# Seven products of halves in place of eight for x times w_in in the last three steps of an attention and two-layer gated kernel

## Chip, cores and metric

The kernel runs on one core of one Trainium2 chip. The metric is device time in microseconds (us), lower is better. The time before is 1128.55 us, the median of 3 runs (1128.35 to 1129.04).

## What is computed

```python
scores = scale * np.matmul(q, k.transpose(0, 1, 3, 2))           # 4 batches x 8 heads, 576 x 64
thresh = np.max(scores, axis=-1, keepdims=True) - tau
scores = np.where(scores >= thresh, scores, -1000000000.0)
attn = softmax(scores)                                           # row max, exp, sum + 1e-9
x = np.matmul(attn, v)  ->  2304 tokens x 512
h = x @ w1_in;  x = (h * clip(h + 3, 0, 6) / 6) @ w1_out         # w_in 512 x 2048, w_out 2048 x 512
h = x @ w2_in;  out = (h / (1 + exp(-1.702 * h))) @ w2_out
```

All arrays are float32. The matmuls run on fp32r operands, each operand split in a high and a low part, and each product is the sum of three: high times high, high times low, low times high.

## The kernel before

The engines are written out by hand, each with its own program and semaphores; nothing schedules them. After the attention the work falls into four steps: step 0 and 1 are the first layer with the first and the second half of the 2048 hidden columns, step 2 and 3 the second layer in the same way. A step 1 or 3 adds to the partial sums that the step before it left in HBM.

Step 0 goes over eight tiles of 288 tokens. The first six are mixed piece by piece into the attention of the next batch (`mixed_piece`); tiles 6 and 7 come behind it (`MIXED` is 6), and this stretch is called the seam below. Steps 1 to 3 go over six tiles of 384 tokens each. A tile has two parts on TensorE (PE):

- `h_chunk` (L526): eight chunks of 128 hidden columns. A chunk sums over `KC` = 4 blocks of 128 rows of w_in, three matmuls a block, so 12 matmuls of 128x384 a chunk and 96 a tile. The chunks go round four PSUM banks (`h_bank`, shown as `mm` and `tr`); chunk c waits until chunk c-4 is read.
- `y_chunk` (L535 in step 1, L537 in steps 2 and 3): the gated h times w_out. Four blocks of 24 matmuls of 128x384 in step 1, three blocks of 24 matmuls of 128x512 in steps 2 and 3, in four other banks (`y_bank`, shown as `score`).

For each h chunk ScalarE (ACT) makes the gate from the bank (L800 Relu of h + 3, or L803 Sigmoid), VectorE (DVE) multiplies it with the bank into `act_f` (L680, L682), ACT rounds that into `g_hi` (L808), and GpSimd (POOL) takes the difference, `g_lo` (L963). For x, ACT makes `x_hi` (L795) and DVE `x_lo` (L672). For the weights of the next step, 512 KB a unit, ACT makes `w_hi` (L787) and POOL `w_lo` (L953); these have two buffers and are made in the tiles of the step before. Every transfer is issued by SyncE (SP), in its own fixed order. At the seam ACT and POOL also split the first eight weight units of step 1 (`SEAM`, `SEAM_SLOTS`).

## Time and profile before

| | |
|---|---|
| median of 3 runs | 1128.55 us |
| the profiled execution | 1127.87 us, span 1126.0 us |
| attention with the first six tiles of step 0 | up to 475.8 us |
| tiles 6 and 7 of step 0 | 475.8 to 526.9 us |
| steps 1, 2, 3 | 526.9 to 726.6, to 924.7, to 1122.9 us |
| busy: PE, DVE, ACT, POOL | 96%, 50%, 49%, 43% |

The page gives busy times and the chain of work that ended last; the trace is asked for groups of instructions, stretches of time and single engines. Durations of one instruction are in ns, times in a stretch in us. Matmuls overlap in the pipeline, so the pace of PE is read from the chain (so many matmuls in so many us), not from the duration of one.

### The profile page before, as it was taken

The page shows a single profiled execution, that of the slowest core. Times are in us where ns is not written, and L with a number is a line of the kernel's source. Part 1 is how long each engine was busy: PE and PEld are TensorE (multiplying, and loading weights), DVE is VectorE, ACT ScalarE, POOL GpSimd, SP SyncE. Part 2 cuts the span into 40 slices and gives each one's busy share as a digit, 9 for nine tenths or more (in the row PEclk, how much of TensorE's full clock was granted, in tenths as well). Part 3 has the DMA queues.
Part 4 walks back from the last instruction along what each step waited for, and adds up shares of the span by engine and source line. Part 5 has one row for each costly group of instructions (what it writes and reads, how often), then busy time and mean ns, then how long its engine had stood idle before and what let it go on. Part 6 is the DMA issues. An engine that isn't in the chain of part 4 may idle for free.

```text
span 1126.0 us, 17711 instructions
## 1 busy us (share of the span) xinstructions
PE 1084.6 (96%) x6720; PEld 1021.7 (91%) x6720; DVE 559.6 (50%) x1040; ACT 549.4 (49%) x1036; POOL 487.7 (43%) x582
## 2 busy tenths in 40 slices
PE   4888899999999999999999999999999999999998
PEld 3676799999999999999999999989999889999987
DVE  5989878887878887433233222223322222332221
ACT  4888876868686866344334322333322223332221
POOL 3566755545545553384544332144333122222222
PEclk9999999999999999999999999999999999999999
DMA  4447453445343622463233322112221101222210
GB/s 123 118 138 187 118 135 109 122 120 140 111 121 87 169 85 78 115 182 127 89 106 122 122 84 84 41 54 94 94 94 57 56 28 57 85 85 84 84 57 28
DMA packets 91044, 112.37 MB, mean 100 GB/s; under 512 B 25536, under 2 KB 69712, under 8 KB 90960
## 3 DMA queue, kind: packets, MB, share of 16 engines
q1 hardware_dynamic: 90656, 110.96, 33.8%
q8 instruction: 53, 0.87, 0.3%
q10 hardware_dynamic: 304, 0.30, 0.1%
q14 instruction: 31, 0.25, 0.1%
HBM read 78.12 MB, written 33.10 MB: 99 GB/s over the span
## 4 chain that ended last, share of the span: by engine, by line
PE 90%; DVE 4%; issue 3%; ACT 2%; DMA 0%; POOL 0%; SPq 0%; ACTq 0%; POOLq 0%
PE mm L526 20%; PE score L537 17%; PE tr L526 14%; PE score L535 12%; PE score L488 7%; PE tr L503 6%; PE mm L535 6%; PE mm L517 6%; DVE prob L648 2%; DVE neg_max L640 1%; DVE pt_lo L666 1%; ACT pt_hi L775 1%; ACT gate L800 0%; DMA q_raw<-in_qT 0%; ACT prob L770 0%
## 5 line engine op out<-in xcount | busy, mean ns | idle before, releaser
L963 POOL TENSOR_TENSOR g_lo<-act_f,g_hi 128x384 fp32r<-128x384 f32 (+1 forms) x208 | 196.5, 950 | 405.2 <-ACT g_hi L808 405.2
L526 PE MATMUL mm<-x_hi,w_hi 128*128 128x384 f32 (+1 forms) x512 | 162.9, 318 | 0.6 <-DVE x_lo L672 0.5
L526 PE MATMUL mm<-x_hi,w_lo 128*128 128x384 f32 (+1 forms) x512 | 162.2, 317 | 0.0
L526 PE MATMUL mm<-x_lo,w_hi 128*128 128x384 f32 (+1 forms) x512 | 162.1, 317 | 0.0
L775 ACT ACTIVATE pt_hi<-tr 128x640 fp32r<-128x640 f32 x144 | 101.7, 706 | 98.3 <-PE tr L503 97.8
L803 ACT ACTIVATE gate<-mm 128x384 f32<-128x384 f32 x48 | 23.7, 494 | 220.6 <-PE mm L526 220.6
L488 PE MATMUL score<-k_hi,q_sp 128*128 128x288 f32 x320 | 97.7, 322 | 29.3 <-DVE prob L648 20.6
L666 DVE TENSOR_TENSOR pt_lo<-tr,pt_hi 128x640 fp32r<-128x640 f32 x144 | 118.1, 820 | 9.8 <-ACT pt_hi L775 8.8
L640 DVE TENSOR_REDUCE neg_max<-score 128x1 f32<-128x576 f32 x144 | 108.2, 752 | 27.4 <-PE score L488 24.3
L933 POOL TENSOR_SCALAR thresh<-neg_max,tau_abs 128x1 f32<-128x1 f32 x144 | 41.6, 289 | 178.6 <-DVE neg_max L640 178.0
L648 DVE SCALAR_TENSOR_TENSOR prob<-score,thresh,prob 128x576 f32<-128x576 f32 x144 | 116.2, 807 | 0.0
L503 PE MATMUL tr<-ident,prob 128*128 128x128 f32 x720 | 105.2, 278 | 7.6 <-issue 5.3
L537 PE MATMUL score<-w_lo,g_hi 128*128 128x512 f32 x288 | 112.3, 390 | 0.0
L537 PE MATMUL score<-w_hi,g_lo 128*128 128x512 f32 x288 | 112.2, 390 | 0.0
L537 PE MATMUL score<-w_hi,g_hi 128*128 128x512 f32 x288 | 112.0, 389 | 0.0
L770 ACT ACTIVATE prob<-score,neg_max 128x576 f32<-128x576 f32 x144 | 106.4, 739 | 7.8 <-DVE neg_max L640 7.5
L808 ACT ACTIVATE g_hi<-act_f 128x384 fp32r<-128x384 f32 (+1 forms) x208 | 102.7, 494 | 7.3 <-DVE act_f L680 4.7
L526 PE MATMUL tr<-x_hi,w_hi 128*128 128x384 f32 (+1 forms) x320 | 105.7, 330 | 0.0
L526 PE MATMUL tr<-x_lo,w_hi 128*128 128x384 f32 (+1 forms) x320 | 105.6, 330 | 0.0
L526 PE MATMUL tr<-x_hi,w_lo 128*128 128x384 f32 (+1 forms) x320 | 105.6, 330 | 0.0
L503 PEld LDWEIGHTS tr<-ident,prob 128*128 128x128 f32 x720 | 83.1, 142 | 18.1 <-issue 17.1
L488 PEld LDWEIGHTS score<-k_hi,q_sp 128*128 128x128 f32 x320 | 62.0, 194 | 40.9 <-DVE prob L648 31.1
(82 smaller groups left out, 2463.6 us busy)
## 6 DMA issues: line engine op xcount, KB each, us to landing
x_raw<-x_t_scratch SPq DMA_DIRECT2D x18, 768.0 KB, 6.3
q_raw<-in_qT SPq DMA_DIRECT2D x64, 144.0 KB, 2.8
k_raw<-in_kT SPq DMA_DIRECT2D x62, 144.0 KB, 2.9
stage<-in_w_in SPq DMA_DIRECT2D x16, 512.0 KB, 7.0
stage<-in_w_out SPq DMA_DIRECT2D x16, 512.0 KB, 5.5
o_parts_scratch<-o_t SPq DMA_DIRECT2D x32, 160.0 KB, 1.8
x_t_scratch<-x_raw SPq DMA_DIRECT2D x8, 576.0 KB, 3.4
part_t_scratch<-y_out SPq DMA_DIRECT2D x8, 576.0 KB, 3.5
```

What stands on the lines that cost most here:

```text
L488: m = pe.matmul(score[:, g % 2, half, 0:HALF], q_sp[:, col:col + P], k_part[:, side, half * HALF:half * HALF + HALF], start=e == 0, stop=e ...
L503: m = pe.transpose(turned_p[:, c * P:c * P + P], prob[:, x % PROBS, c * P:c * P + P], ident[:, :])
L526: m = pe.matmul(bank[:, 0:width], w[:, col:col + P], x[:, k, 0:width], start=(k == 0 and e == 0), stop=(k == KC - 1 and e == 2))
L535: r = pe.matmul(bank[:, 0:width], w[:, col + m * P:col + m * P + P], g[:, c, 0:width], **ends)
L537: r = pe.matmul(bank[:, :], g[:, c, m * P:m * P + P], w[:, col:col + DM], **ends)
L640: dve.tensor_reduce(neg_max[:, r:r + 1], score[:, g % 2, :, 0:HALF], AX.XY, ALU.max, negate=True).then_inc(max_done, 1)
L648: dve.scalar_tensor_tensor(out=p, in0=score[:, g % 2, :, 0:HALF], scalar=thresh[:, r:r + 1], in1=p, op0=ALU.is_ge, op1=ALU.mult, accum_out ...
L666: dve.tensor_tensor(pt_place(pt_lo, x), turned_place(x), pt_place(pt_hi, x), ALU.subtract).then_inc(pt_lo_done, 1)
L770: act.activation(prob[:, g % PROBS, 0:S].rearrange("p (a n) -> p a n", a=2), score[:, g % 2, :, 0:HALF], ACT.Exp, bias=neg_max[:, r:r + 1] ...
L775: act.activation(pt_place(pt_hi, x), turned_place(x), ACT.Copy).then_inc(pt_hi_done, 1)
L808: act.activation(g_hi[:, c, 0:width], act_f[:, c % 2, 0:width], ACT.Copy).then_inc(g_hi_done, 1)
L963: pool.tensor_tensor(g_lo[:, c, 0:width], act_f[:, c % 2, 0:width], g_hi[:, c, 0:width], ALU.subtract).then_inc(g_lo_done, 1)
```

## The change

Attention and step 0 keep their instructions. In steps 1 to 3, two tiles of 384 tokens are taken together as a pair (three pairs a step, `d` = 0 to 8). The pair's x is cut in halves by token and by row of w_in, w_in in halves by row and by column, and the four quarters of h are formed from seven products of such halves or of their sums and differences (`PRODUCT`), where the plain way has eight. One product is 6 matmuls of 128x384 (two blocks of 128 rows, three each). The hidden columns of a step go in four groups of two chunks (n and n + 4), so a group is seven products and gives four quarters ("items" C11, C12, C21, C22), and the products go round six banks (`p_bank`).

The four items of a group are summed from the seven banks: ACT copies the first product into `sum12`, and DVE adds the other six in seven additions, each with one operand in SBUF and one in a bank, into `sum11`, `sum12`, `sum21`, `sum22`. ACT makes the gate from the sum into a ring of three places (`act_ring`), DVE multiplies it in place with the sum (both in SBUF, `gate_item`), ACT rounds (`high_item`), POOL subtracts (`low_item`). An ACT gate waits until POOL is done with the item three before it.

The sums of halves of x (4 pieces a pair) are made and split on DVE and ACT behind a pair's products, for the next pair (`bring`). The sums of halves of w_in (8 units a step) are made and split on DVE, ACT and POOL behind the products of a step's last pair, for the next step. w_out has one buffer now; its eight chunks are split in a step's first pair, two behind the first item of each of its four groups, by ACT (`high_out_unit`) and POOL (`low_out_unit`). The second part keeps its matmuls; its blocks run over the two tiles of a pair, the first three blocks leave out the last group until all three have the other groups (`dense_block`). SP loads x in pieces of 192 columns, w_in in rows of 128 columns, and stores and loads y by block. The first w_in units of step 1, their sums included, are made at the seam. SBUF places are given by hand, and buffers of the attention are reused.

```diff
+    PAIR_TILES = NTOK // (2 * TT)
+    DENSE = (STEPS - 1) * PAIR_TILES
+    HIGH_A = ("A11", "A22", "A12", "S3", "S2", "S1", "S4")
+    HIGH_B = ("B11", "B22", "B21", "T3", "T1", "T2", "T4")
+    PRODUCT = {1: ("A11", "B11"), 2: ("A12", "B21"), 3: ("S4", "B22"), 4: ("A22", "T4"), 5: ("S1", "T1"),
+               6: ("S2", "T2"), 7: ("S3", "T3")}
+    PRODUCT_ORDER = (1, 2, 6, 7, 5, 3, 4)
+    GROUPS = FC // 2
+    PRODUCTS = GROUPS * len(PRODUCT_ORDER)
+    BANKS = 6
...
+    ITEMS = [(0, "C11")]
+    for n in range(1, GROUPS):
+        ITEMS += [(n - 1, "C22"), (n - 1, "C12"), (n - 1, "C21"), (n, "C11")]
+    ITEMS += [(GROUPS - 1, "C22"), (GROUPS - 1, "C12"), (GROUPS - 1, "C21")]
...
+        def coming(d):
+            if d + 1 == DENSE:
+                return []
+            x = [("x", 4 * max(d + 1, 0) + i) for i in range(4)]
+            units = unit_of(1, 0, 0) if d < 0 else next_units(d)
+            if units is None:
+                return [x[0:2], x[2:4]]
+            w = [("w", units + i) for i in range(2 * GROUPS)]
+            if d < 0:
+                return [x[2:4], w[4:6], w[6:8]] if d == -1 else [w[2:4]]
+            return [x[0:2], w[0:2], x[2:4], w[2:4], w[4:6], w[6:8]]
+        def emptied_behind(d):
+            if d < 0:
+                return [1, 2, 3]
+            if next_units(d) is None:
+                return [3, 5] if blocks_y(d) == 8 else [2, 4]
+            return [0, 2, 4, 5, 6, 7] if blocks_y(d) == 8 else [0, 1, 3, 4, 5, 5]
...
+            def product(d, n, k):
+                p = PRODUCT_ORDER[k]
+                a, b = HIGH_A.index(PRODUCT[p][0]), HIGH_B.index(PRODUCT[p][1])
+                bank = p_bank[(len(PRODUCT_ORDER) * n + k) % BANKS][:, 0:TT]
+                for j in range(2):
+                    for e, (w, x) in enumerate(((ws_hi, xs_hi), (ws_hi, xs_lo), (ws_lo, xs_hi))):
+                        m = pe.matmul(bank, w[:, n, j, b, :], x[j][:, a, :], start=j == 0 and e == 0, stop=j == 1 and e == 2)
+                m.then_inc(made, 1)
...
+            def bank_free(d, n, k):
+                at = len(PRODUCT_ORDER) * n + k
+                if at >= BANKS:
+                    m, i = divmod(at - BANKS, len(PRODUCT_ORDER))
+                    if i == 0:
+                        pe.wait_ge(p1_copied, GROUPS * d + m + 1)
+                    else:
+                        pe.wait_ge(evicted, 6 * (GROUPS * d + m) + i)
...
+            for d in range(DENSE):
+                for n in range(GROUPS):
+                    units_split(pe, dense_step(d), 0, n)
+                    if n == 0:
+                        pe.wait_ge(pair_split, 4 * (d + 1))
+                    for k in range(len(PRODUCT_ORDER)):
+                        bank_free(d, n, k)
+                        product(d, n, k)
+                for b in range(3):
+                    dense_block(d, b, 0, GROUPS - 1)
+                for b in range(3):
+                    dense_block(d, b, GROUPS - 1, GROUPS)
+                for b in range(3, blocks_y(d)):
+                    dense_block(d, b, 0, GROUPS)
...
+            def pair_sums(q):
+                a21, a11, a22, a12 = (pair_raw[:, q % 2, i, :] for i in range(4))
+                dve.wait_ge(pair_lo_done, q + 1)
+                dve.tensor_tensor(a22, a21, a22, ALU.add).then_inc(pair_s1_done, 1)
+                dve.tensor_tensor(a21, a11, a21, ALU.subtract).then_inc(pair_s1_done, 1)
+                dve.wait_ge(pair_s1_done, 3 * q + 2)
+                dve.tensor_tensor(a11, a22, a11, ALU.subtract).then_inc(pair_s1_done, 1)
+                dve.wait_ge(pair_s1_done, 3 * q + 3)
+                dve.tensor_tensor(a12, a12, a11, ALU.subtract).then_inc(pair_sums_done, 1)
...
+            def gate_item(d, n, which, bank):
+                k = item(d, n, which)
+                place = act_ring[:, k % 3, :]
+                dve.wait_ge(gate_done, k + 1)
+                if dense_step(d) == 1:
+                    r = dve.scalar_tensor_tensor(out=place, in0=place, scalar=6.0, in1=bank, op0=ALU.min, op1=ALU.mult)
+                else:
+                    r = dve.tensor_tensor(place, place, bank, ALU.mult)
+                r.then_inc(gated_done, 1)
+            def evict(d, n, k):
+                dve.wait_ge(made, PRODUCTS * d + len(PRODUCT_ORDER) * n + k + 1)
+                return p_bank[(len(PRODUCT_ORDER) * n + k) % BANKS][:, 0:TT]
+            def add_c11(d, n):
+                bank = evict(d, n, 1)
+                dve.wait_ge(p1_copied, GROUPS * d + n + 1)
+                dve.tensor_tensor(sum11[:, :], sum12[:, n % 2, :], bank, ALU.add).then_inc(evicted, 1)
+            def add_u2(d, n):
+                place = sum12[:, n % 2, :]
+                dve.tensor_tensor(place, place, evict(d, n, 2), ALU.add).then_inc(evicted, 1)
+            def add_u3(d, n):
+                bank = evict(d, n, 3)
+                dve.wait_ge(evicted, 6 * (GROUPS * d + n) + 2)
+                dve.tensor_tensor(sum21[:, :], sum12[:, n % 2, :], bank, ALU.add).then_inc(evicted, 1)
+            def add_c22_u4(d, n):
+                bank, place = evict(d, n, 4), sum12[:, n % 2, :]
+                dve.wait_ge(evicted, 6 * (GROUPS * d + n) + 3)
+                dve.tensor_tensor(sum22[:, :], sum21[:, :], bank, ALU.add).then_inc(c22_added, 1)
+                dve.tensor_tensor(place, place, bank, ALU.add).then_inc(evicted, 1)
+            def add_c12(d, n):
+                bank, place = evict(d, n, 5), sum12[:, n % 2, :]
+                dve.wait_ge(evicted, 6 * (GROUPS * d + n) + 4)
+                dve.tensor_tensor(place, place, bank, ALU.add).then_inc(evicted, 1)
+            def add_c21(d, n):
+                dve.tensor_tensor(sum21[:, :], sum21[:, :], evict(d, n, 6), ALU.add).then_inc(evicted, 1)
...
+            for d in range(DENSE):
+                first_of_step = d % PAIR_TILES == 0
+                for n in range(GROUPS + 1):
+                    if n > 0:
+                        gate_item(d, n - 1, "C22", sum22[:, :])
+                        gate_item(d, n - 1, "C12", sum12[:, (n - 1) % 2, :])
+                        gate_item(d, n - 1, "C21", sum21[:, :])
+                    if n < GROUPS:
+                        add_c11(d, n)
+                        add_u2(d, n)
+                        gate_item(d, n, "C11", sum11[:, :])
+                        add_u3(d, n)
+                        add_c22_u4(d, n)
+                        add_c12(d, n)
+                        add_c21(d, n)
+                empty = 0
+                for two, many in zip(coming(d), emptied_behind(d)):
+                    bring(two)
+                    if two[0][0] == "x":
+                        bring_low(two)
+                    while empty < many:
+                        empty_block(d, empty)
+                        empty += 1
+                    if two[0][0] == "w":
+                        bring_low(two)
+                for b in range(empty, blocks_y(d)):
+                    empty_block(d, b)
...
+            for d in range(DENSE):
+                first_of_step = d % PAIR_TILES == 0
+                for n in range(GROUPS + 1):
+                    if n > 0:
+                        act.wait_ge(evicted, 6 * (GROUPS * d + n - 1) + 5)
+                        gate_of(d, n - 1, "C12", sum12[:, (n - 1) % 2, :])
+                        act.wait_ge(evicted, 6 * (GROUPS * d + n))
+                        gate_of(d, n - 1, "C21", sum21[:, :])
+                    if n < GROUPS:
+                        copy_p1(d, n)
+                    if n > 0:
+                        high_item(d, n - 1, "C22")
+                        high_item(d, n - 1, "C12")
+                    if n < GROUPS:
+                        act.wait_ge(evicted, 6 * (GROUPS * d + n) + 1)
+                        gate_of(d, n, "C11", sum11[:, :])
+                    if n > 0:
+                        high_item(d, n - 1, "C21")
+                    if n < GROUPS:
+                        high_item(d, n, "C11")
+                        if first_of_step:
+                            high_out_unit(dense_step(d), 2 * n)
+                            high_out_unit(dense_step(d), 2 * n + 1)
+                        act.wait_ge(c22_added, GROUPS * d + n + 1)
+                        gate_of(d, n, "C22", sum22[:, :])
+                for two in coming(d):
+                    bring(two)
...
+            for d in range(DENSE):
+                if d == 0:
+                    pool.wait_ge(y_stored, 16 * TILES)
+                for k in range(len(ITEMS)):
+                    low_item(d, k)
+                    if d % PAIR_TILES == 0 and k % 4 == 0 and k < 4 * GROUPS:
+                        low_out_unit(dense_step(d), k // 2)
+                        low_out_unit(dense_step(d), k // 2 + 1)
+                for two in coming(d):
+                    bring(two)
```

The first place is DVE's program in a group of a pair (step 1): before, for four chunks of a tile, and now, for four items. In the names, sum_104 is sum11, sum_106 sum12, sum_103 sum21, sum_105 sum22.

```order
L680 SCALAR_TENSOR_TENSOR act_f<-gate,mm 128x384 [waits g_lo_done,gate_done] x2
L680 SCALAR_TENSOR_TENSOR act_f<-gate,tr 128x384 [waits g_lo_done,gate_done] x2
```

```order
L1038 SCALAR_TENSOR_TENSOR act_ring<-act_ring,sum_105 128x384 [waits gate_done]
L1038 SCALAR_TENSOR_TENSOR act_ring<-act_ring,sum_106 128x384 [waits gate_done]
L1038 SCALAR_TENSOR_TENSOR act_ring<-act_ring,sum_103 128x384 [waits gate_done]
L1051 TENSOR_TENSOR sum_104<-sum_106,tr 128x384 [waits p1_copied,made]
L1055 TENSOR_TENSOR sum_106<-sum_106,score 128x384 [waits made]
L1038 SCALAR_TENSOR_TENSOR act_ring<-act_ring,sum_104 128x384 [waits gate_done]
L1060 TENSOR_TENSOR sum_103<-sum_106,score 128x384 [waits evicted,made]
L1065 TENSOR_TENSOR sum_105<-sum_103,score 128x384 [waits evicted,made]
L1066 TENSOR_TENSOR sum_106<-sum_106,score 128x384
L1071 TENSOR_TENSOR sum_106<-sum_106,mm 128x384 [waits evicted,made]
L1074 TENSOR_TENSOR sum_103<-sum_103,mm 128x384 [waits made]
```

Four instructions became eleven, and the multiplication with the gate of C11 stands ahead of the additions that free the next banks.

The second place is POOL's program at the start of step 1: before, the splits of the last seam units between the first tile's g_lo, and now, the first pair's items and chunks of w_out.

```order
L963 TENSOR_TENSOR g_lo<-act_f,g_hi 128x384 [waits g_hi_done] x4
L953 TENSOR_TENSOR w_lo<-stage,w_hi 128x512 [waits w_hi_done] x4
L963 TENSOR_TENSOR g_lo<-act_f,g_hi 128x384 [waits g_hi_done] x8
```

```order
L1530 TENSOR_TENSOR gd_lo<-act_ring,gd_hi 128x384 [waits g_hi_done,y_stored]
L1522 TENSOR_TENSOR wo_lo<-unit_raw_89,wo_hi 128x512 [waits wo_hi_done]
L1522 TENSOR_TENSOR wo_lo<-unit_raw_90,wo_hi 128x512 [waits wo_hi_done]
L1530 TENSOR_TENSOR gd_lo<-act_ring,gd_hi 128x384 [waits g_hi_done] x4
L1522 TENSOR_TENSOR wo_lo<-unit_raw_89,wo_hi 128x512 [waits wo_hi_done]
```

Two splits of w_out stand between the items of each of the first pair's groups, and the very first item waits for the last store of step 0.

The third place is ACT's program at the start of tile 6, at the seam: before, and now.

```order
L787 ACTIVATE w_hi<-stage 128x1024 [waits pt_lo_done,inv_stored1,pv_done,inv_stored0,stage_loaded0,o_stored1,o_stored0]
L787 ACTIVATE w_hi<-stage 128x1024 [waits stage_loaded1]
L800 ACTIVATE gate<-mm,three 128x288 [waits mm_filled] x2
```

```order
L1263 ACTIVATE ws_hi<-unit_raw_89 128x384 [waits pt_lo_done,inv_stored1,pv_done,inv_stored0,unit_loaded0,o_stored1,o_stored0]
L1268 ACTIVATE ws_hi<-unit_raw_89 128x512 [waits unit_sums_done]
L1263 ACTIVATE ws_hi<-unit_raw_90 128x384 [waits unit_loaded1]
L1268 ACTIVATE ws_hi<-unit_raw_90 128x512 [waits unit_sums_done]
L1236 ACTIVATE gate<-mm,three 128x288 [waits mm_filled] x2
```

Ahead of tile 6's first gates, ACT now twice waits for sums that DVE makes behind a split on POOL.

## Rows read from the trace of the kernel before

**Rows 1.** The page: busy time of the engines, clock granted to PE by slice

```profile
PE 1084.6 (96%) x6720; PEld 1021.7 (91%) x6720; DVE 559.6 (50%) x1040; ACT 549.4 (49%) x1036; POOL 487.7 (43%) x582
...
PEclk9999999999999999999999999999999999999999
```

**Rows 2.** Stretches: seam, steps 1, 2, 3; length, busy by engine, clock, DMA

```profile
460.47:527.00 66.53, 66.46 (x504) 66.02 (x503) 21.18 (x43) 25.80 (x54) 39.76 (x43) 1.00 0.47 134
527.00:726.58 199.58, 199.58 (x1153) 199.58 (x1152) 55.28 (x96) 69.40 (x131) 74.49 (x68) 1.00 0.28 97
726.58:924.71 198.13, 198.13 (x1009) 181.04 (x1009) 55.14 (x90) 61.68 (x128) 69.94 (x64) 1.00 0.21 70
924.71:1126.00 201.29, 198.16 (x1009) 180.73 (x1007) 53.25 (x87) 52.43 (x116) 48.44 (x48) 1.00 0.22 71
```

**Rows 3.** The chain that ended last, steps 1 and 2: start, us, what

```profile
597.62 4.16 PE tr L526 x24
...
610.10 16.64 PE score L535 x96
...
743.22 16.36 PE score L537 x72
759.58 4.18 PE mm L526 x24
```

**Rows 4.** Groups by shape, DVE and ACT: busy us, mean ns, idle before

```profile
L682 DVE TENSOR_TENSOR act_f<-gate,mm 128x384 f32<-128x384 f32 x48 | 26.6, 554 | 78.3 <-ACT gate L803 78.3
...
L635 DVE TENSOR_TENSOR k_lo<-k_raw,k_hi 128x576 fp32r<-128x576 f32 x1 | 0.8, 758 | 0.0
...
L803 ACT ACTIVATE gate<-mm 128x384 f32<-128x384 f32 x48 | 23.7, 494 | 220.6 <-PE mm L526 220.6
...
L800 ACT ACTIVATE gate<-mm,three 128x384 f32<-128x384 f32 x24 | 14.0, 582 | 99.5 <-PE mm L526 99.4
...
L808 ACT ACTIVATE g_hi<-act_f 128x384 fp32r<-128x384 f32 x144 | 74.8, 519 | 4.0 <-DVE act_f L682 2.5 <-DVE act_f L680 1.5
```

**Rows 5.** Groups by shape, POOL

```profile
L963 POOL TENSOR_TENSOR g_lo<-act_f,g_hi 128x384 fp32r<-128x384 f32 x144 | 145.2, 1014 | 382.2 <-ACT g_hi L808 382.2
...
L953 POOL TENSOR_TENSOR w_lo<-stage,w_hi 128x512 fp32r<-128x512 f32 x64 | 83.6, 1330 | 18.4 <-ACT w_hi L787 18.4
```

**Rows 6.** All x_lo on DVE, both inputs in SBUF: min/median/max ns

```profile
L672 DVE TENSOR_TENSOR x_lo<-x_raw,x_hi x104: 435/547/1312, 113.2 to 1077.8; 128x384 fp32r<-128x384 f32 x72, 128x288 fp32r<-128x288 f32 x32
```

**Rows 7.** One such x_lo run and the POOL work beside it, in order of time

```profile
645.59 2.72 DVE L672 TENSOR_TENSOR x_lo<-x_raw,x_hi 128x384 fp32r<-128x384 f32 x4 [1.01 <-ACT x_hi L795]
...
644.49 1.99 POOL L963 TENSOR_TENSOR g_lo<-act_f,g_hi 128x384 fp32r<-128x384 f32 x2 [1.06 <-ACT g_hi L808]
```

**Rows 8.** The seam in order of time: chain, then ACT, DVE, POOL

```profile
475.78 3.40 PE mm L526 x24
...
501.51 3.16 PE mm L526 x24
...
477.79 1.06 ACT L787 ACTIVATE w_hi<-stage 128x1024 fp32r<-128x1024 f32 x1 [2.65 <-DMA stage<-in_w_in]
...
479.97 0.88 ACT L800 ACTIVATE gate<-mm,three 128x288 f32<-128x288 f32 x2
...
480.48 0.85 DVE L680 SCALAR_TENSOR_TENSOR act_f<-gate,mm 128x288 f32<-128x288 f32 x2 [4.28 <-ACT gate L800]
...
478.92 5.05 POOL L953 TENSOR_TENSOR w_lo<-stage,w_hi 128x512 fp32r<-128x512 f32 x4 [4.26 <-ACT w_hi L787]
```

**Rows 9.** DMA issues: count, KB each, median us to landing

```profile
part_t_scratch<-y_out SPq DMA_DIRECT2D x8, 576.0 KB, 3.5
...
v_raw<-in_v SPq DMA_DIRECT2D x32, 128.0 KB, 2.2
```

**Rows 10.** The end of the chain

```profile
1106.51 16.38 PE score L537 x72
...
1122.91 0.69 DVE L695 SCALAR_TENSOR_TENSOR y_out<-score,part 128x512 f32<-128x512 f32 x1 [4.75 <-PE score L537]
```

769 lines of the change are left out of this document (540 added, 229 removed).

## The prediction

> **What bounds the kernel now.** The page comes first: PE is busy 96% of the span, no other engine over 50%, and the clock granted to PE stands at the top of its tenths in every slice [rows 1]. The stretches say where the rest is: from the seam on, PE is busy 66.46 of 66.53, 199.58 of 199.58 and 198.13 of 198.13 us, and in the last step all but the 3 us of the end; the clock is 1.00 there, the level of 2.4 GHz, and DVE, ACT and POOL are busy a quarter to a third [rows 2]. Busy time alone would not prove a bound, since matmuls overlap; the chain does: in steps 1 to 3 it is PE and nothing else, 24 matmuls of 128x384 in 4.16 us, 96 in 16.64, and 72 of 128x512 in 16.36 [rows 3]. So a 128x384 matmul costs 4.16 / 24 = 0.173 us on the path, and whatever PE need not do there comes off, as long as the others keep pace. The idle time ahead of ACT's and DVE's groups is their slack [rows 4].
>
> **What is taken away.** A pair of tiles had 2 x 96 = 192 matmuls for h. It now has 4 groups x 7 products x 6 = 168. That is 24 a pair, 216 in nine pairs, x 0.173 = **37.4 us** off the path. The second part keeps its 192 matmuls of 128x384 or 144 of 128x512 a pair. Everything else only adds work to other engines, and the question is where PE waits for it.
>
> **An ordinary group.** PE makes seven products in 42 x 0.173 = 7.28 us. DVE now has eleven instructions in that time: seven additions with one operand in a bank, which I price like the multiplication with a bank, 0.554 us [rows 4], 3.9 us together; and four multiplications with both inputs in SBUF, nearest x_lo of the same width, median 0.547 [rows 6], 2.2 us. That is 6.1 of 7.28. ACT has four gates (0.582 in step 1, 0.494 later), four roundings of 0.519 and a copy from a bank, about 0.5: 4.9 us at most [rows 4]. POOL has four subtractions of 1.014, 4.1 us [rows 5]. All fit as sums. They also form a ring, since the third gate after an item waits until POOL is through with that item. I walk it from DVE's multiplication of C22. ACT is first busy with the gate of C21 and the copy of the next group's first product, then rounds C22 (0.58 + 0.5 + 0.52 = 1.6 us). POOL subtracts C22 (to 2.6). ACT makes the gate of the next C11 (to 3.2). DVE's multiplication of C11 now meets POOL's next subtraction. Such a meeting is in the trace: the x_lo that begins while POOL works takes up to 1.31 us in place of 0.547, and the run of four at 645.59 begins under the g_lo pair that started at 644.49 [rows 6, 7]; it ends about 0.4 after POOL's instruction. So C11 is done at 2.6 + 1.0 + 0.4 = 4.0, five additions of 0.554 follow, and the round closes at 6.8 us. PE needs 7.28, so it sets the pace. The margin of 0.5 us a group is thin, but lateness is buffered: a bank is wanted again only six products later, so its reader may be some 4 us late before PE stops, and the second part of the pair, 33 us, resets the count. Cost: nothing; if it fails, every group pays.
>
> **The first pair of a step.** Two chunks of w_out a group add two splits on ACT, about 0.6 each (between the 0.519 of 384 and the twice as wide 1.06 of L787) [rows 4, 8], and two on POOL of 1.33 [rows 5]. POOL then has 4 x 1.014 + 2 x 1.33 = 6.7 us, and where it gives way to DVE's four multiplications another 4 x 0.4: 8.3 against 7.28, so it falls behind by 1.0 us a group in the three later groups, 3 us in all. The banks bear that (4 us), and the last group's items are wanted only 9.4 us after the last product, because the first three blocks do 54 other matmuls first. Nothing in steps 2 and 3. In the first pair of step 1, POOL's first item also waits for the last store of step 0 (3.5 us for 576 KB [rows 9], begun only after DVE has read tile 7's last block), so two or three us more are missing and the buffer is about used up: I take 1 us, with 0 and 4 as ends.
>
> **Behind the products.** The coming pair's x wants, of DVE, four pieces of a difference of 576, four sums of 192 and a difference of 768. From 0.547 for 384 and 0.758 for 576 [rows 4, 6] I estimate 0.35 for 192 and 0.96 for 768, so about 3.1 us a piece and, with ACT's roundings between, 7 us for two; 14 of the 33 us of the second part. In the last pair of a step eight units of w_in come on top, in four rounds of ACT 0.5, POOL 2 x 1.0, DVE about 1.1, ACT 0.6, some 4.6 us each, 18 in all. With 3.3 us until DVE is free this is 36 us in a stretch of 33, so DVE comes about 3 us late to the next step's banks. PE does not see it: the first bank that DVE must empty is wanted one group, 7 us, later, and the last units are used in the third and fourth group only. Cost: nothing, with 0 and 4 us at each of two borders as ends. SP's loads between are small against these times: 128 KB lands in 2.2 us [rows 9].
>
> **The seam.** Before, ACT rounded two units of 1.06 us, made the first gates of tile 6 at 479.97, DVE read the first banks at 480.48, and PE, which began tile 6 at 475.78, lost 0.24 us on its first 24 matmuls (3.40 against 3.16) [rows 8]. Chunk 4 wants the first bank at 475.78 + 4 x 1.58 = 482.1. Now ACT goes through two units in a row: round, wait for POOL (1.0), for DVE's sums (1.1), round 0.6, and POOL puts another 1.3 between. That is 3.2 us for the first unit and 4.0 for the second, begun about half a us before PE begins tile 6 (its last x must be rounded first), so the gate falls at about 482.5 and the bank is free at 483.4: 1.3 us of standstill. In tile 7, DVE and ACT put the first half of x between the gates; the last g_lo then comes about 1.5 us behind its use. Together 3 us, with 0 (all of it buffered) and 8 (each of these waits seen in full, and tile 7 late with its x) as ends. The end of the program is as before: one block of 512 and its store [rows 10].
>
> **The sum.** 1127.87 - 37.4 + 3 + 1 = 1094.5 for the profiled execution. That one stands 0.7 us under the median of the three runs, so against the median it is **1095 us**. Its own range is 1091 (all hidden) to 1100.
>
> **Rivals.**
> - *POOL and the port in first pairs.* The 1.0 us a group is not buffered but paid in all four groups of three pairs: 12 us more, 1107. For it: 8.3 against 7.28, and multiplications that wait make POOL wait in turn. Against it: the six banks and the 9.4 us. Chance 0.15.
> - *The borders of steps are late.* The 3 us overrun grows to 7 and DVE's first additions stop PE, or the second half of x is not split in time: 4 us twice, 1103. For it: long hand-to-hand chains over three engines. Against it: units are only wanted group by group. Chance 0.10.
> - *The seven products cost more than their matmuls.* Each ends with a semaphore and a change of bank. If each cost what separates 24 matmuls of 4.18 us behind a block from 4.16, 0.02 us, 252 products would cost 5 us: 1100. The change of bank every 12 matmuls costs nothing in the chain now [rows 3]. Chance 0.05.
> - *Slower: DVE and POOL shut each other out in every group.* The x_lo that meets POOL loses 1.31 - 0.55 = 0.76 us [rows 6]. My walk counts one such meeting a group. If all four multiplications met one, the round would be 6.8 + 3 x 0.76 = 9.1 us, 1.8 over PE's 7.28, in 36 groups 65 us: about 1160. It turns the sign when a round passes 7.28 + 33.4 / 36 = 8.2 us. Against it: three of the four come when POOL has run dry in an ordinary group. The Trainium skill (SBUF — State Buffer, section on the two separate sides) has this as a rule: a DVE instruction with two SBUF inputs and a GpSimd instruction hold one shared pair of ports in turn, each for its whole length. By that rule the trace agrees with its 1.31 us, additions with an operand in a bank stay free, as the constant 0.554 suggests, and the price is that of the meetings only. Chance 0.07.
>
> **Chances.** Forecast 0.62, the rivals 0.15, 0.10, 0.05 and 0.07, and 0.01 for something that ends near the old time. A measurement of this kernel can tell about 0.2%, 2.3 us, from no change. Faster by more than that: 0.92; within it 0.01; slower 0.07. The range of 1090.5 to 1108 takes in the forecast and the three rivals on its side, about nine in ten; I leave the slow side out.
>
> **What would show it.** PE: 1512 matmuls of products in place of 1728, at 0.173 us each, pairs of about 62 us; 24 fewer in each. Waits of PE in the trace: a few us between 482 and 540, next to none later. DVE's additions at 0.55; multiplications of C11 near 1.0 and the other three near 0.55 in ordinary groups, longer in first pairs. POOL without idle time in the first pair of each step. The forecast is wrong if the chain of steps 2 and 3 holds DVE, ACT or POOL by more than 1%, or if a group of products in an ordinary pair takes over 7.4 us.

## The result, and the profile after

| | |
|---|---|
| before | 1128.45 us, median of 4 runs (1126.59 to 1129.04) |
| after | 1117.64 us, median of 4 runs (1116.64 to 1119.27) |
| ratio | 0.9909, 95% interval 0.9893 to 0.9925 |
| profiled execution after | 1117.04 us, span 1115.2 us |

The change makes the kernel faster by 0.9%. The forecast was 1095 us, the range 1090.5 to 1108: the direction was right, the size was not, and the time lies outside the range.

The busy line of the page, as in [rows 1]:

```profile
PE 1057.3 (95%) x6504; PEld 988.0 (89%) x6504; DVE 824.0 (74%) x1543; ACT 609.3 (55%) x1120; POOL 513.5 (46%) x595
```

PE issues 6504 matmuls, 216 fewer than before: what was to be taken away is gone. But its share fell from 96% to 95%, so PE now waits. The chain that ended last says the same: before, it was PE for 90% of the span and DVE for 4%, and now:

```profile
PE 70%; DVE 14%; issue 5%; ACT 5%; POOL 2%; DMA 2%; SPq 1%; ACTq 0%; DVEq 0%; POOLq 0%
```

The stretches of after, from the same point of the seam on, with the columns of [rows 2] (length; busy of PE, weight loads, DVE, ACT, POOL; clock; DMA):

```profile
460.47:537.24 76.77, 71.19 (x508) 68.85 (x507) 41.71 (x86) 30.08 (x63) 38.77 (x42) 0.98 0.42 114
537.24:729.00 191.76, 188.76 (x1083) 186.92 (x1081) 142.20 (x264) 85.82 (x156) 75.37 (x68) 1.00 0.32 96
729.00:920.97 191.97, 187.04 (x938) 168.25 (x938) 144.23 (x259) 83.10 (x157) 77.48 (x68) 1.00 0.24 73
920.97:1115.20 194.23, 187.92 (x937) 169.63 (x935) 121.07 (x212) 70.79 (x138) 67.25 (x60) 0.99 0.25 79
```

Step 1 begins at 537.24 in place of 526.72, and the later stretches have 3.0, 4.9 and 6.3 us in which PE is not busy (of the last, some 3 us are the end of the program, as before). Smaller stretches, cut where PE's products and blocks begin, say where. The first row is the products of step 2's first pair, then its blocks, then the products of the next pair, then those of step 3's first pair:

```profile
729.00:764.63 35.63, 30.70 (x169) 28.87 (x169) 30.81 (x48) 19.84 (x39) 24.71 (x21) 1.00 0.27 78
764.63:797.31 32.68, 32.68 (x145) 27.03 (x145) 22.93 (x41) 11.40 (x19) 9.31 (x8) 1.00 0.29 93
797.31:826.46 29.15, 29.15 (x170) 29.14 (x168) 21.95 (x41) 15.10 (x32) 13.41 (x13) 1.00 0.12 37
...
920.97:955.50 34.53, 31.43 (x170) 30.45 (x169) 30.03 (x48) 18.71 (x39) 24.35 (x21) 0.95 0.30 96
```

An ordinary pair makes the 168 matmuls of its products in 29.15 us, 0.1735 each, and its blocks run in 32.68 without a wait. All six ordinary pairs are like it (products in 29.12 or 29.15, blocks in 33.28 in step 1 and 32.68 later), and the blocks of first pairs run without a wait too. The chain there is PE alone, as in [rows 3]:

```profile
797.47 2.10 PE mm L797 x12
799.58 1.04 PE tr L797 x6
800.62 3.12 PE score L797 x18
```

What is missing lies in four places:

| place | length | without waits | lost |
|---|---|---|---|
| up to step 1's first product | 537.24 | 526.72 (before) | 10.5 |
| products, first pair of step 1 | 33.65 | 29.15 | 4.5 |
| the same of step 2 | 35.63 | 29.15 | 6.5 |
| the same of step 3 | 34.53 | 29.15 | 5.4 |

37.4 - 10.5 - 16.4 = 10.5 us, and the spans differ by 1126.0 - 1115.2 = 10.8.

What PE waited for in the first pair of step 2 (us in total, times, longest; where the text gives a stop by the starts of two matmuls, it is 0.17 us longer than the wait, since it takes in the matmul ahead of it):

```profile
PE mm L797 <- ACT sum L1303: 2.3, 2, 1.5
PE tr L797 <- DVE sum L1051: 1.5, 1, 1.5
PE score L797 <- DVE sum L1051: 0.5, 1, 0.5
PE mm L797 <- DVE y_ring L1087: 0.5, 1, 0.5
```

None of the four names a transfer or POOL. All are DVE or ACT coming late to a bank (`y_ring` is DVE emptying a block of the step before). The order of time on DVE shows why, from 2.9 us before the step begins at 729.00 (start, us, instruction, and in brackets idle time and what ended it):

```profile
726.09 1.09 DVE L1003 TENSOR_TENSOR unit_raw<-unit_raw 128x128 f32<-128x128 f32 x1 [0.91 <-POOL ws_lo L1502]
...
728.80 1.41 DVE L1008 TENSOR_TENSOR unit_raw<-unit_raw 128x128 f32<-128x128 f32 x1
730.13 0.55 DVE L1087 SCALAR_TENSOR_TENSOR y_ring<-mm,y_ring 128x384 f32<-128x384 f32 x1
730.90 0.69 DVE L1013 TENSOR_TENSOR ws_lo<-unit_raw,ws_hi 128x512 fp32r<-128x512 f32 x1 [0.23 <-ACT ws_hi L1268]
732.50 1.09 DVE L1003 TENSOR_TENSOR unit_raw<-unit_raw 128x128 f32<-128x128 f32 x1 [0.90 <-POOL ws_lo L1502]
...
738.38 0.54 DVE L1051 TENSOR_TENSOR sum<-sum,mm 128x384 f32<-128x384 f32 x1
```

and on POOL beside it:

```profile
724.94 2.09 POOL L1502 TENSOR_TENSOR ws_lo<-unit_raw,ws_hi 128x384 fp32r<-128x384 f32 x2 [1.30 <-ACT ws_hi L1263]
728.77 1.29 POOL L1508 TENSOR_TENSOR ws_lo<-unit_raw,ws_hi 128x512 fp32r<-128x512 f32 x1 [1.75 <-ACT ws_hi L1268]
```

A round for two units of w_in goes from 726.09 to 732.50: 6.4 us. In each, two of DVE's sums that take 0.28 alone meet a POOL instruction: one takes 1.09, ending 0.15 us behind POOL's second L1502, and the other takes 1.41 beside POOL's low part of the even unit's sums. DVE's first addition of the new step (L1051) is at 738.38, 9.4 us after PE began it. PE had filled all six banks by 736.0.

On ACT, two more things stand in line:

```profile
736.64 0.63 ACT L1268 ACTIVATE ws_hi<-unit_raw 128x512 fp32r<-128x512 f32 x1 [1.53 <-DVE unit_raw L1008]
737.18 0.47 ACT L1303 ACTIVATE sum<-mm 128x384 f32<-128x384 f32 x1
737.67 1.28 ACT L1313 ACT_TABLE_LOAD   x1
...
743.34 1.33 ACT L1277 ACTIVATE wo_hi<-unit_raw 128x512 fp32r<-128x512 f32 x2 [2.70 <-DMA unit_raw<-in_w_out]
```

The copy of the first product stands behind the last round (PE's 1.5 us), and ACT then waits 2.70 us for w_out. In SP's order that load stands behind the store of the last block, which DVE empties only behind the last round (at 738.46); SP issues the load at 738.86.

In the first pair of step 1 it is the same: two rounds of 6.4 us for the last four units of the seam, and DVE's first addition at 545.82, 8.6 us after the products began.

In the seam, set against [rows 2, 8], PE's parts of tiles 6 and 7 have grown. Tile 6 begins 1.06 us later, its h takes 15.06 in place of 12.84, its y 12.84 for 12.73, tile 7's h 15.67 for 12.64 and its y 16.83 for 12.73: together 10.5 us. The waits from tile 6 on:

```profile
PE mm L756 <- DVE act_f L967: 3.1, 3, 1.9
PE score L763 <- POOL g_lo L1497: 1.4, 3, 0.8
PE tr L756 <- DVE act_f L967: 0.9, 1, 0.9
```

Part of the growth is clock. These are the last 15 us before step 1:

```profile
521.90:537.24 15.34, 13.96 (x88) 12.93 (x87) 12.02 (x26) 6.13 (x11) 7.43 (x7) 0.89 0.41 125
```

A mean clock of 0.89 over 15.34 us costs 0.11 x 15.34 = 1.7 us. It fell behind PE's waits for g_lo: from 525.0 to 528.4 the matmuls of 288 columns stand 0.240 us apart in place of 0.133. The 0.95 in the first pair of step 3 is the same (0.05 x 34.53 = 1.7 us), behind a stop of 2.9 us at 930.13: from 932.1 to 934.7 the matmuls stand 0.32 us apart in place of 0.173, the lower of the clock's two levels (1.2 and 2.4 GHz).

### The profile page after: what moved, and what is told of

Read it like the earlier page. It is cut to its first block, busy times and chain, and to the rows that moved or that the text cites. A ratio compares the mean times of both kernels' runs of the same rounds, so it can differ in the third digit from the quotient of the medians.

```text
span 1115.2 us, 18294 instructions
## 1 busy us (share of the span) xinstructions
PE 1057.3 (95%) x6504; PEld 988.0 (89%) x6504; DVE 824.0 (74%) x1543; ACT 609.3 (55%) x1120; POOL 513.5 (46%) x595
## 4 chain that ended last, share of the span: by engine, by line
PE 70%; DVE 14%; issue 5%; ACT 5%; POOL 2%; DMA 2%; SPq 1%; ACTq 0%; DVEq 0%; POOLq 0%
PE score L836 10%; PE score L797 8%; PE score L718 8%; PE mm L756 6%; PE mm L797 6%; PE tr L733 6%; PE mm L763 6%; PE mm L747 6%; PE tr L836 5%; PE tr L797 3%; PE score L834 3%; DVE prob L939 2%; DVE unit_raw L1008 2%; PE tr L834 1%; PE mm L834 1%
## 5 line engine op out<-in xcount | busy, mean ns | idle before, releaser
L1530 POOL TENSOR_TENSOR gd_lo<-act_ring,gd_hi 128x384 fp32r<-128x384 f32 x144 | 155.8, 1103 | 278.0 <-ACT gd_hi L1319 271.0
L718 PE MATMUL score<-k_lo,q_sp 128*128 128x288 f32 x320 | 91.9, 302 | 0.0
L1319 ACT ACTIVATE gd_hi<-act_ring 128x384 fp32r<-128x384 f32 x144 | 72.1, 520 | 29.3 <-DVE act_ring L1040 20.8
L797 PE MATMUL score<-xs_hi,ws_hi 128*128 128x384 f32 x234 | 78.7, 336 | 3.2 <-DVE sum L1051 1.7
L797 PE MATMUL score<-xs_hi,ws_lo 128*128 128x384 f32 x234 | 78.2, 334 | 0.0
L797 PE MATMUL score<-xs_lo,ws_hi 128*128 128x384 f32 x234 | 78.2, 334 | 0.0
L836 PE MATMUL score<-wo_hi,gd_hi 128*128 128x512 f32 x192 | 74.7, 389 | 0.0
L836 PE MATMUL score<-wo_hi,gd_lo 128*128 128x512 f32 x192 | 74.7, 389 | 0.0
L836 PE MATMUL score<-wo_lo,gd_hi 128*128 128x512 f32 x192 | 74.7, 389 | 0.0
L1040 DVE TENSOR_TENSOR act_ring<-act_ring,sum 128x384 f32<-128x384 f32 x96 | 68.2, 751 | 5.2 <-ACT act_ring L1313 4.1
```

Source lines behind the costliest of these rows:

```text
L718: m = pe.matmul(score[:, g % 2, half, 0:HALF], q_sp[:, col:col + P], k_part[:, side, half * HALF:half * HALF + HALF], start=e == 0, stop=e ...
L797: m = pe.matmul(bank, w[:, n, j, b, :], x[j][:, a, :], start=j == 0 and e == 0, stop=j == 1 and e == 2)
L836: r = pe.matmul(bank, g[:, u, c, m * P:m * P + P], w[:, c, :], **ends)
L1319: act.activation(gd_hi[:, u, c, :], act_ring[:, k % 3, :], ACT.Copy).then_inc(g_hi_done, 1)
L1530: pool.tensor_tensor(gd_lo[:, u, c, :], act_ring[:, g % 3, :], gd_hi[:, u, c, :], ALU.subtract).then_inc(g_lo_done, 1)
```

## The experiments

**Theories.** *Late preparation*: DVE and ACT come too late out of the rounds for w_in, and all waits of first pairs follow from that, lengthened by collisions of DVE and POOL. *Pace*: in first pairs the splits of w_out make a group slower than PE's 7.28 us, whatever came before (this was the forecast's first rival). For the seam: two units in a row ahead of the first gates, or too little engine time in any order. Each experiment was timed beside the kernel before, whose median lay between 1127.2 and 1128.0 us; the ratios are to it, with 95% intervals in brackets. The intervals of e5, e7 and e8 overlap with e3's, f2's with f1's, f3's with f2's, and those of e2 and e4 with after's: the medians alone do not settle such pairs, and the reading rests on the stretches of the traces. All times of stretches are of one profiled execution each.

### e1: steps 2 and 3 without preparing w_in

```diff
+        def absent(unit):
+            step, i = 1 + unit // STEP_UNITS, unit % STEP_UNITS
+            return step > 1 and i < 2 * GROUPS
```

(`load_late_unit`, `uses` and the waits leave such units out, and `coming` gives x alone.)

> Steps 2 and 3 use the w_in parts of step 1 (output differs): the eight units of w_in are neither loaded nor split nor summed behind the last pair of steps 1 and 2; w_out is still split. The changed kernel's first pairs of steps 2 and 3 take 35.6 and 34.5 us for their products where 29.1 are free of waits: 11.9 us lost. Theory 'late preparation': DVE, ACT and POOL come 9 us late out of the rounds for w_in, the w_out work then starts behind that, and all of the 11.9 us has this root: both first pairs at 29.1 to 30, total about 1106. Rival 'pace of the w_out splits' (a group at 8.05 us whatever came before): only the first stalls of each (2.4 us at step 2, 2.9 plus the 1.8 us of low clock at step 3) go, 4 to 5 us remain: total about 1110.5.

Measured: 1104.33 us, ratio 0.9795 (0.9773 to 0.9817), 13.3 us under after. The first pairs of steps 2 and 3:

```profile
726.89:756.01 29.12, 29.12 (x169) 29.12 (x169) 23.76 (x39) 19.38 (x39) 21.13 (x19) 1.00 0.33 99
912.35:941.50 29.15, 29.15 (x170) 29.15 (x169) 23.90 (x40) 18.11 (x38) 21.14 (x19) 1.00 0.40 129
```

No wait is left, though POOL splits w_out as before: 11.9 us. (The other 1.4 of the 13.3 is not explained by the edit. The traces differ by more than that ahead of the seam: in after, e1, e2, e3, e5, e6 and e7, which have the same instructions up to there, tile 6 begins at anything from 474.7 to 477.0 us.) Late preparation is the root. The pace is real all the same. These are DVE's additions of C11, one a group, in e1's first pair of step 2:

```profile
729.17 0.55 DVE L1059 TENSOR_TENSOR sum<-sum,mm 128x384 f32<-128x384 f32 x1 [1.52 <-PE mm L805]
...
736.67 0.54 DVE L1059 TENSOR_TENSOR sum<-sum,tr 128x384 f32<-128x384 f32 x1
...
744.65 0.54 DVE L1059 TENSOR_TENSOR sum<-sum,score 128x384 f32<-128x384 f32 x1
...
753.30 0.54 DVE L1059 TENSOR_TENSOR sum<-sum,score 128x384 f32<-128x384 f32 x1
```

Groups of 7.5, 8.0 and 8.7 us where PE needs 7.28: DVE falls back 2.3 us, and six banks bear it, as the prediction had it. They can't bear 9 us of lateness as well.

### e2: steps 2 and 3 without preparing w_out

The same edit with `i >= 2 * GROUPS`, and `high_out_unit` and `low_out_unit` only in step 1's first pair (`d == 0`).

> Steps 2 and 3 use the w_out parts of step 1 (output differs): no chunk of w_out is loaded or split in their first pairs; w_in is still prepared behind the last pairs. Theory 'late preparation': the stalls at the start of the first pairs stay (2.4 us at step 2, 2.9 plus 1.8 at step 3) and the later ones go since nothing else is slow: 33.3 and 34 us less 3.3 and 0.4, total about 1114. Rival 'pace of the w_out splits': nearly all of the 11.9 us goes, total about 1107. If both theories share it, e1 and e2 each save more than their own part, and the savings add to over 11.9.

Measured: 1113.61 us, ratio 0.9878 (0.9849 to 0.9907), 4.0 us under after. The pairs take 32.00 and 32.57 us; the first:

```profile
729.83:761.83 32.00, 29.93 (x169) 29.00 (x169) 27.34 (x53) 18.11 (x37) 17.24 (x17) 1.00 0.16 50
```

The waits at the start of each pair stay (0.70 and 1.65 us, and 2.89), those behind them go. They lose 2.9 and 3.4 us, 6.3 together. So of after's 11.9 us some 6.3 need only the lateness. Of the other 5.6, 1.7 are the clock, which fell in after and not in e2 behind a stop of the same length; whether w_out has a part in that is not shown. Some 3.9 need both, late engines and w_out's part: without lateness (e1) they are not there either.

### e3: the low part of the even units' sums on DVE at the borders

```diff
-                    elif i % 2:
+                    elif i % 2 or i >= STEP_UNITS:
                         low_unit_sums(i)
...
-                    if what == "w" and i % 2 == 0:
+                    if what == "w" and i % 2 == 0 and i < STEP_UNITS:
```

> The low part of the sums of the even w_in units of steps 2 and 3 is made by DVE (0.7 us each) in place of POOL (1.29). Same arithmetic. Theory 'collisions of DVE and POOL lengthen the rounds' (a sum of 1.09 in place of 0.28, a last low part of 1.41 in place of 0.29 in each round of 6.4 us): the second collision goes, POOL is free for the next units earlier, a round falls to about 5.3 us, DVE comes 4 to 5 us earlier to the step, and the total falls by 3 to 5 us to about 1113. Rival 'the round is a chain of hand-overs, DVE only gets more work': round stays at 6.2 to 6.8 us, total 1117 to 1119.

Measured: 1110.54 us, ratio 0.9848 (0.9828 to 0.9869), 7.1 us under after, more than expected. A round on DVE:

```profile
725.37 1.09 DVE L1003 TENSOR_TENSOR unit_raw<-unit_raw 128x128 f32<-128x128 f32 x1 [0.91 <-POOL ws_lo L1502]
...
728.08 0.29 DVE L1008 TENSOR_TENSOR unit_raw<-unit_raw 128x128 f32<-128x128 f32 x1
728.29 0.55 DVE L1087 SCALAR_TENSOR_TENSOR y_ring<-mm,y_ring 128x384 f32<-128x384 f32 x1
728.76 1.28 DVE L1013 TENSOR_TENSOR ws_lo<-unit_raw,ws_hi 128x512 fp32r<-128x512 f32 x2
730.94 1.08 DVE L1003 TENSOR_TENSOR unit_raw<-unit_raw 128x128 f32<-128x128 f32 x1 [0.90 <-POOL ws_lo L1502]
```

L1008 is back at 0.29, the round takes 5.57 us in place of 6.41, and the first pairs of steps 2 and 3 32.20 and 31.74 (of what the second gains, 1.7 us are the clock, which does not fall here). DVE does 0.68 us more a round and the round is 0.84 shorter: the collision, not the work, was the cost, and it lay on the chain, since ACT's last rounding waits for that sum and the next round's for ACT.

### e4: only one unit ahead of the first gates

```diff
-    SEAM_SLOTS = {END - 3: 0, END - 1: 1}
+    SEAM_SLOTS = {END - 3: 0}
...
-                return [x[2:4], w[4:6], w[6:8]] if d == -1 else [w[2:4]]
+                return [x[2:4], w[4:6], w[6:8]] if d == -1 else [w[1:2], w[2:4]]
```

> Unit 1 of step 1's w_in is prepared behind the gates of tile 6 in place of the last slot of the attention; unit 0 stays. Same arithmetic. Theory 'two units in a row hold up the first gates': the stall of 2.07 us at 485.4 goes, and the seam is 1.5 to 2 us shorter unless tile 7 pays it back; total about 1115.5. Rival 'the seam is short of DVE and ACT as a whole': the work comes back in tile 7 (stalls at 512 to 526 grow by as much), total 1117 to 1119.

Measured: 1119.57 us, ratio 0.9930 (0.9910 to 0.9951): a miss for the first theory as a gain. Its longest wait at the seam:

```profile
PE mm L756 <- DVE act_f L967: 4.1, 1, 4.1
```

Tile 6's h takes 12.86 us, free of the stall, and tile 7's 19.70 in place of 15.67, at a mean clock of 0.83. From tile 6's first matmul to step 1's the two kernels take the same: 60.5 us, and 60.4 in after. The stall did come from the units; moved work only stalls the next tile.

### e5 to e8: one more edit each

e5 is e3 with `low_late_unit` on DVE at the borders.

```diff
                     if what == "x":
                         low_pair(i)
+                    elif i >= STEP_UNITS:
+                        low_late_unit(i)
```

> As e3, and the low part of the raw w_in halves of steps 2 and 3 is made by DVE too; POOL does nothing at the borders. In e3 a round took 5.58 us: POOL's two instructions (1.38 and 1.02), then DVE 4.2 us with one of its sums held up to 1.09 (in place of 0.28). Theory 'DVE and POOL take turns, so a round costs the sum of both': DVE's own work is 2.3 + 1.4 + 2 x 0.55 + one block of 0.55 = 5.3 us and nothing collides, round 5.2 to 5.5, total 0 to 2 us under e3 (1109 to 1110.5). Rival 'POOL's work is mostly beside DVE's' : the round grows by 1.1 to 6.2 and more, total 2 to 4 us over e3.

Measured: 1107.80 us, ratio 0.9830 (0.9814 to 0.9846), 2.7 under e3. Its rounds:

```profile
722.67 1.02 DVE L1001 TENSOR_TENSOR ws_lo<-unit_raw,ws_hi 128x384 fp32r<-128x384 f32 x2
723.61 0.28 DVE L1009 TENSOR_TENSOR unit_raw<-unit_raw 128x128 f32<-128x128 f32 x1
...
726.19 1.28 DVE L1019 TENSOR_TENSOR ws_lo<-unit_raw,ws_hi 128x512 fp32r<-128x512 f32 x2
727.39 0.55 DVE L1001 TENSOR_TENSOR ws_lo<-unit_raw,ws_hi 128x384 fp32r<-128x384 f32 x1
```

4.72 us from 722.67 to 727.39, without a gap: DVE alone is faster than DVE and POOL together were (6.41). The first pairs of steps 2 and 3 take 30.28 and 29.94 us. I had expected 5.2 to 5.5; instructions in a row overlap by some 0.1 us each, which I had not taken off.

e6 is e3 with w_out's low part on DVE.

```diff
                         add_c21(d, n)
+                        if first_of_step:
+                            low_out_unit(dense_step(d), 2 * n)
+                            low_out_unit(dense_step(d), 2 * n + 1)
```

> As e3, and the low part of w_out is made by DVE (about 0.7 us each) behind the last addition of a group, in place of POOL (1.3 to 1.6). Theory 'POOL and its collisions set the 8.05 us of a group in the first pairs': a group falls to 7.5 us or less and the stalls inside the first pairs of steps 1 to 3 (e3: 0.5 to 1.1 us at the fourth group) go; total 2 to 3 us under e3, about 1108. Rival 'ACT and w_out's transfers set them': stalls at the second group (1.70 at 746.4 in e3) stay, total as e3 within 1 us; if DVE, then 7.5 us a group over PE's 7.28, costs more than it saves, over e3.

Measured: 1106.27 us, ratio 0.9813 (0.9798 to 0.9828), 4.3 under e3; first pairs of steps 2 and 3 30.59 and 30.41 us, 2.9 less than in e3. Of e3's three waits in step 2 (0.38, 1.70, 0.69 us) one of 0.70 is left, and the later groups take 7.6 to 7.7 us in place of 8.0: POOL and its meetings did set the pace.

e7 is e3 with the first chunk of w_out loaded earlier.

```diff
                     if b == 2 and units is not None:
                         load_late_unit(units + 7)
+                        load_late_unit(units + 8)
                 if units is not None:
-                    load_late_unit(units + 8)
```

> As e3, and the first chunk of w_out is loaded behind the third block in place of behind the last. Theory 'ACT stands still for w_out's transfer' (1.89 us at 740.6 in e3, whence the late gates): the 1.70 us stall of PE at 746.4 shrinks by a half or more, total 1 to 2 us under e3. Rival 'POOL's pace sets it anyway': the stall stays, same as e3 within 0.7 us.

Measured: 1110.41 us, ratio 0.9842 (0.9820 to 0.9865), the same as e3. In its trace the 1.70 us stall fell to 0.51 but the last one rose from 0.69 to 1.08, and the two pairs are 0.9 and 1.1 us shorter, less than these medians can show. Whether the load is worth anything by itself stays open.

e8 is e3 with that edit for step 1's units too, so also at the seam.

> The e3 edit for all units, those of step 1 at the seam included. Theory 'the seam too loses by collisions of POOL's low parts with DVE': the stall of 2.1 to 2.5 us at 485 shrinks by about 0.6, the later ones by 1 to 2 in sum, total 1 to 3 us under e3. Rival 'the seam is short of DVE time' : DVE has more to do, total at or over e3, first product at 538 or later.

Measured: 1108.66 us, ratio 0.9829 (0.9815 to 0.9844), 1.9 under e3. Tile 7's h takes 14.55 us (15.67 in after), and the first pair of step 1 31.52 (33.39 in e3). The stop at tile 6's first bank, which the theory had shrink, is as in after: 2.1 us.

### f1: e5 to e8 together, and f2: the seam's x spread

> The edits of e5, e6, e7 and e8 together: low parts of the w_in sums by DVE everywhere, of the raw w_in halves by DVE at the borders, of w_out by DVE in first pairs, the first chunk of w_out loaded earlier. Theory 'they remove different waits (a border's rounds, the pace of the first pair, ACT's wait for w_out)': first pairs of steps 2 and 3 at 29.2 to 29.8 us, of step 1 at 31 to 33, total 1103 to 1105. Rival 'DVE becomes the bound of the first pairs and borders (7.5 us a group over 7.28)': first pairs stay at 30 to 31 us, total 1106 to 1108.

Measured: 1100.53 us, ratio 0.9761 (0.9747 to 0.9774). First pairs of steps 1 and 2:

```profile
535.83:566.14 30.31, 30.05 (x171) 28.85 (x170) 25.54 (x53) 18.09 (x35) 11.91 (x12) 1.00 0.34 104
724.22:753.34 29.12, 29.12 (x170) 29.12 (x170) 25.89 (x54) 19.35 (x39) 12.06 (x12) 1.00 0.29 91
```

Step 3's takes 29.14. The borders of steps 2 and 3 now cost nothing. DVE's first addition of step 2 is at 728.07, 3.9 us after the products began: lateness of 4 us is free, 9.4 us was not. The separate gains over e3 (2.7, 4.3, 0.1, 1.9) sum to 9.0 and together give 10.0, which is the same within the intervals.

```diff
-                    if ti > MIXED and c == 2:
-                        pair_sums(0)
-                        pair_sums(1)
+                    if ti > MIXED and c == 2:
+                        pair_sums(0)
+                    if ti > MIXED and c == 3:
+                        pair_sums(1)
```

(f2; `low_pair` at c = 0 and 1, `low_pair_sums` at 4 and 5, ACT's at 3 and 4.)

> As f1, and in tile 7 the work on the first half of x stands one piece behind each of six gates in place of two pieces behind every second (DVE), and one behind each of two (ACT). Theory 'the seam's stalls in tile 7 (0.5 to 0.9, 1.03 and some 2.5 us in the first block of y) come from two pieces in a row between gates': 1 to 3 us under f1. Rival 'DVE, ACT and POOL have too little time there in any order': same as f1 within 0.7 us.

Measured: 1099.20 us, ratio 0.9746 (0.9733 to 0.9760), 1.3 under f1. From tile 6's first matmul to step 1's it takes 55.80 us, f1 59.69: 3.9 less. Only 1.4 of that is tile 7's h (13.15 us in place of 14.57), where the edit is; 0.7 lies in tile 6, which the edit leaves alone, and 1.7 in tile 7's y, where the clock fell in f1 (0.90) and not in f2 (1.00). The first pair of step 1 gives 2.2 back (32.55): DVE and ACT are late there.

### f3: both early units at once, and f4: the price of x

```diff
-                    high_late_unit(SEAM_SLOTS[g])
-                    high_unit_sums(SEAM_SLOTS[g])
+                    high_late_unit(0)
+                    high_late_unit(1)
+                    high_unit_sums(0)
+                    high_unit_sums(1)
```

(f3, on f2; likewise on DVE and POOL, with `SEAM_SLOTS = {END - 1: 0}`.)

> As f2, and the first two units of w_in are made together in the attention's last slot: ACT rounds both, POOL subtracts both, DVE sums both, ACT rounds both sums, in place of one whole chain after the other. In f2 the chains run from 477.2 to 484.0, 3.4 us each, and the first gate stands behind them. Theory 'the first gates are late by the hand-overs of two chains in a row': the gate comes 1.5 us earlier, the stall of 1.27 us at 485.2 (2.0 in f1) goes, total 1 to 1.5 us under f2. Rival 'it is the bulk of the work or the transfer of the unit (landed at 477.1)': same as f2 within 0.5 us.

Measured: 1097.62 us, ratio 0.9729 (0.9714 to 0.9744). The fastest kernel of the study, 20.0 us under after and 30 under before. Both tiles' h are clean (13.02 and 12.80 us), and what is left of the seam's loss lies in tile 7's y (second line):

```profile
502.80:515.60 12.80, 12.80 (x98) 12.80 (x97) 11.81 (x28) 6.32 (x13) 4.95 (x6) 1.00 0.12 33
515.60:532.53 16.93, 15.36 (x99) 14.42 (x97) 13.58 (x29) 8.43 (x17) 6.62 (x7) 0.90 0.37 113
```

Of its 4.2 us over 12.73, the clock of 0.90 is 1.7 and waits for g_lo are 1.6.

f4 is f2 with the first half of x made behind all gates of tile 7.

> As f2, but the first half of x for the first pair is made behind all of tile 7's gates. It is no improvement but a price: theory 'the waits left in tile 7 (0.24, 0.46, and 1.8 us in the first block of y) come from the x work between its gates': they go, and PE stands instead, some 3 to 7 us, before the first product, since x is complete 7 us later; total 2 to 6 us over f2. Rival 'they come from something else (tile 7's gates themselves, POOL)': the waits in tile 7 stay, and the standstill before the first product is added.

Measured: 1105.37 us, ratio 0.9801 (0.9785 to 0.9816), 6.2 over f2. The waits from tile 7 on:

```profile
PE mm L797 <- DVE xs_lo L995: 5.2, 1, 5.2
...
PE score L763 <- POOL g_lo L1514: 0.6, 1, 0.6
```

The waits inside tile 7 nearly go, and PE stands 5.2 us for x; the first pair of step 1 then takes 35.7 us, at a clock of 0.92, in place of 32.55. So the x work does cause them, and behind the gates is no better place for it.

## Why the prediction was wrong

Two steps failed: the price of a round for w_in behind the products, and the reckoning of the first pair and of the lateness ahead of it as if each had the banks for itself.

*What is taken away*: right. 216 matmuls fewer at 0.1733 us, 37.4 us; pairs of 62.4 and 61.8 us.

*An ordinary group*: right in its result, and on the safe side in its walk. Additions took 0.55 us as priced. The meeting of the C11 multiplication with POOL is there in three groups of four, but dearer in the forecast (done in 1.4 us, "near 1.0") than in the trace, 0.74 against 0.55:

```profile
806.84 4.26 POOL L1530 TENSOR_TENSOR gd_lo<-act_ring,gd_hi 128x384 fp32r<-128x384 f32 x4 [3.50 <-ACT gd_hi L1319]
808.50 0.74 DVE L1040 TENSOR_TENSOR act_ring<-act_ring,sum 128x384 f32<-128x384 f32 x1
```

These are all multiplications of an ordinary pair and of a first one (min, median, max in ns):

```profile
L1040 DVE TENSOR_TENSOR act_ring<-act_ring,sum x13: 551/552/742, 801.1 to 823.1; 128x384 f32<-128x384 f32 x13
...
L1040 DVE TENSOR_TENSOR act_ring<-act_ring,sum x12: 559/1152/1648, 739.5 to 763.3; 128x384 f32<-128x384 f32 x12
```

The slower case, that DVE and POOL shut each other out in every group, did not come: with PE setting the pace, three of four multiplications fall into POOL's gaps (ten of the thirteen take 0.55). Products cost no overhead for their semaphores: 0.1735 us a matmul.

*The first pair of a step*: the pace was right (8.3 us a group forecast, 8.05 between DVE's last additions of C11 in after, 7.5 to 8.7 in e1) and so was "the banks bear that" if taken alone (e1: no wait). The total of 1 us was wrong, 16.4 us measured, because this step of the reckoning spent the same 4 us of bank buffer that the next one, on what comes behind the products, also counted on. POOL's wait for the last store, the forecast's reason for step 1, is there (its first item begins at 548.83), but PE's waits in that pair name only DVE and ACT, and the first and longest of them names DVE, which comes 8.6 us late.

*Behind the products*: this step failed. "Some 4.6 us each" for a round of w_in was 6.4. (The parts that it lists make only 4.2 us, and 3.3 + 14 + 18 make 35.3, not 36; without its two meetings the measured round would be about 4.5, so 4.6 was a good price for a round that meets nobody.) Its working had only durations of instructions that meet nobody, although the walk of the ordinary group had priced a meeting; here two of DVE's sums a round met POOL, 0.8 and 1.1 us, on a chain with no slack (e3 takes one of them out and the round falls by 0.84 us, e5 both and it is 4.72). Four rounds too long by 1.8 make 7 us, and DVE was 9.4 us behind the step's begin, not "about 3". "Cost: nothing" would have held for the 3: f1, 3.9 us late, loses nothing. The rival of late borders had the mechanism, 4 us for each of two, and was too small (6.5 and 5.4) because it counted only DVE's first additions and the second half of x: ACT late at the gates, w_out's load behind the last unit (2.70 us) and the slow group add to them (about 3.9 us, by e2), and after a stop of 2.9 us the clock fell (1.7).

*The seam*: right in the first mechanism (PE stops for the first bank, forecast 1.3 us until 483.4, measured 2.1 until 485.4) and too small as a whole, 3 for 10.5; 8 had been given as an end. The work on x between tile 7's gates was priced at 1.5 us behind one g_lo; tile 7's h came out 3.0 us longer and its y 4.1, of it 1.7 by the clock. Of the 3.0, POOL's low part of the w_in sums makes about 1.1 (e8) and x, two pieces at a time, 1.4 (f2). Of the medians, f2 and f3 win back 1.3 and 1.6 us.

The seam, the first pair of step 1 (4.5 where 1 was taken) and the two borders (11.9 where 0 was taken) make 10.5 + 4.5 + 11.9 - 4 = 22.9 us, which takes 1094.5 to 1117.4; the profiled execution took 1117.04. Of the prediction's own signs, "next to none later" is false: PE waits in the first pairs of steps 2 and 3. The chain of these two steps (from 729 us on) holds DVE's L1008 by 2.6%, L1040 by 2.5% and w_out's transfer by 1.6%, over the 1% that was to show the forecast wrong. POOL was not without idle time in first pairs (busy 24.71 of 35.63 us in step 2's). A group of an ordinary pair over 7.4 us did not occur.
